# Attention and two feed-forward layers on one core: sums of pv, weight stores, key/query preparations and weight splits at other places of their slots, and four landing buffers for the second layer's weights

## What is computed

```python
scores = q @ k.T / 8                    # 4 batches, 8 heads, 576 positions, dimension 64
attn = softmax(scores, only the 32 largest of each row kept)
x = (attn @ v), laid out as 2304 tokens x 512
h = x @ w_in;   g = h if h >= 1, 0 if h <= -1, else (h + 1)**2 / 4;   x = g @ w_out   # layer 1
h = x @ w_in2;  out = (relu(h) ** 2) @ w_out2                                        # layer 2
```

## Time and profile before

| what | value |
|---|---|
| median of three runs | 1256.47 us |
| the profiled execution | 1258.67 us |
| its span | 1256.9 us |
| TensorE busy | 1191.6 us (95%) |
| VectorE, ScalarE, GpSimd busy | 850.7, 799.0, 745.1 us |
| mean granted TensorE clock | 0.978 of 2.4 GHz |

### The profile page before, as it was taken

One profiled execution on the slowest core, in us unless ns is written; L12 is line 12 of the kernel. 1 busy time (PEld: TensorE's weight loads), 2 busy tenths in 40 slices (PEclk: granted clock), 3 DMA queues, 4 the chain that ended last, 5 costly groups with the idle time before them and its releaser, 6 DMA issues.

```text
span 1256.9 us, 24445 instructions
## 1 busy us (share of the span) xinstructions
PE 1191.6 (95%) x8760; PEld 1128.9 (90%) x8760; DVE 850.7 (68%) x1884; ACT 799.0 (64%) x1788; POOL 745.1 (59%) x620
## 2 busy tenths in 40 slices
PE   6787899999989999999999999999999999999998
PEld 3676889998889999999999999999999999999997
DVE  7999899999888799999999987868730111110000
ACT  7887666776656676776767665666554665554443
POOL 6767787768877767767766766656652222222222
PEclk9958999999999999999999999999999999999999
DMA  6765978567879943244358831456349300870000
GB/s 246 281 246 209 350 274 300 195 249 261 289 267 364 390 153 106 100 136 142 127 168 306 291 126 41 146 178 207 104 147 368 147 35 4 310 290 18 18 17 17
DMA packets 94920, 239.53 MB, mean 191 GB/s; under 512 B 7760, under 2 KB 46672, under 8 KB 82512
## 3 DMA queue, kind: packets, MB, share of 16 engines
q1 hardware_dynamic: 94800, 237.98, 53.2%
HBM read 166.12 MB, written 71.83 MB: 189 GB/s over the span
## 4 chain that ended last, share of the span: by engine, by line
PE 72%; POOL 10%; DVE 6%; ACT 5%; issue 4%; DMA 1%; SPq 1%; ACTq 0%; POOLq 0%
PE h_ps L613 21%; PE y_ps L634 14%; PE y_ps L628 13%; PE score_ps L613 6%; PE pv_ps L572 6%; PE tr_ps L545 4%; POOL s_sb L1087 3%; PE score_ps L510 3%; POOL prob L1092 3%; DVE top L920 2%; DVE rest L922 2%; POOL kq_lo L1070 2%; POOL w_out L1078 1%; PE pv_ps L584 1%; POOL g_lo L1105 1%
## 5 line engine op out<-in xcount | busy, mean ns | idle before, releaser
L1105 POOL TENSOR_TENSOR g_lo<-rg,g_hi 128x256 fp32r<-128x256 f32 x288 | 213.5, 741 | 438.3 <-ACT g_hi L823 231.8
L613 PE MATMUL h_ps<-xt_hi,w_in 128*128 128x256 f32 x1880 | 392.9, 292 | 1.5 <-ACT rg L810 0.9
L613 PEld LDWEIGHTS h_ps<-xt_hi,w_in 128*128 128x128 f32 x1880 | 311.3, 192 | 3.6 <-ACT rg L810 1.1
L920 DVE MAX8 top<-rest 128x8 f32<-128x576 f32 x432 | 304.4, 745 | 0.4
L613 PE MATMUL h_ps<-xt_lo,w_in 128*128 128x256 f32 x940 | 267.1, 284 | 0.0
L1087 POOL TENSOR_SCALAR s_sb<-s_sb,top 128x576 f32<-128x576 f32 x126 | 224.9, 1785 | 16.6 <-DVE top L920 16.6
L628 PE MATMUL y_ps<-g_hi,w_out 128*128 128x256 f32 x1152 | 231.7, 284 | 1.0 <-ACT ys L789 0.7
L922 DVE MATCH_REPLACE8 rest<-top,rest 128x576 f32<-128x576 f32 x288 | 211.5, 741 | 0.0
L634 PE MATMUL y_ps<-w_out,g_hi 128*128 128x512 f32 x576 | 203.6, 395 | 3.8 <-DVE w_out L1004 3.1
L1092 POOL TENSOR_TENSOR prob<-s_sb,prob 128x576 f32<-128x576 f32 x128 | 183.4, 1435 | 14.7 <-ACT s_sb L749 3.9
L628 PEld LDWEIGHTS y_ps<-g_hi,w_out 128*128 128x128 f32 x1152 | 189.6, 192 | 2.2 <-issue 1.0
(11 more groups left out here) (90 smaller groups left out, 2077.0 us busy)
## 6 DMA issues: line engine op xcount, KB each, us to landing
w_in<-w_scratch SPq DMA_DIRECT2D x32, 1024.0 KB, 6.8
w_out<-w_scratch SPq DMA_DIRECT2D x32, 1024.0 KB, 8.1
ks<-kq_scratch SPq DMA_DIRECT2D x46, 576.0 KB, 6.1
qs<-kq_scratch SPq DMA_DIRECT2D x152, 128.0 KB, 4.2
w_scratch<-w_in SPq DMA_DIRECT2D x16, 1024.0 KB, 8.4
w_scratch<-w_out SPq DMA_DIRECT2D x16, 1024.0 KB, 8.3
v_sb<-in_vv_dram SPq DMA_DIRECT2D x48, 325.0 KB, 6.0
stage<-in_w_dram SPq DMA_DIRECT2D x24, 512.0 KB, 4.7
```

What stands on the lines that cost most here:

```text
L613: last = pe.matmul(h_bank(k), wi[:, f // 2, w, m, cols], x[:, m, :], start=(m == 0 and n == 0), stop=(m == KT - 1 and n == 2))
L920: dve.max(best, src[:, :]).then_inc(rank_step, 1)
L1105: pool.tensor_tensor(g_lo[k % 2][:, :], g_sb[k % 2][:, :], g_hi[k % 2][:, :].bitcast(F32), ALU.subtract).then_inc(g_lo_done, 1)
```

## The change

It edits where things stand in their slots, and the landing buffers:

- The sums of pv stand two operations late in slots 4 to 8 too (`n < SIGNED`, which is 9).
- Preparations: slot 10 becomes 9, 17 becomes 18, and 28, 30, 32 become 29, 31, 33. For slots 10 to 17 (`SINGLE`; these are 12 and 15) ScalarE's kq_hi stands at the head of its slot.
- Layer 1's blocks are stored in slots 10 to 20 instead of 10 to 17.
- Layer 2's blocks: slots 19 to 28 take 1, 1, 1, 2, 2, 2, 2, 2, 2, 1 of them (before: 1, 2, 2, 1, 2, 2, 1, 2, 2, 1). ScalarE's high part stands at the head of the slot (`split_second`), VectorE's low part behind op 2 and activate(3n). Block 17 goes from VectorE to GpSimd, where the low part stands at the slot's end as before.
- Landing: four buffers, `stage[0]`, `stage[1]`, and the idle kq_lo and kq_hi. Block i is loaded when block i - 4 is split. The kq buffers are taken after the restack of the ninth preparation (slot 18), and the tenth (slot 29) waits until all 32 blocks are split.
- In slots 18 to 22 (`DEFERRED`) activate(3n + 2) goes behind both(0) of the next slot. From slot 18 on activate(3n + 1) stands in front of op 4 instead of behind it.
- ScalarE's `hi_at(q)` stands behind the exponential of t = 1 in every slot.

```diff
--- before.py
+++ after.py
@@ -32,17 +32,20 @@
 SIGNED = 9
 PREPS = BATCH * PAIRS
 PREP_ORDER = (2, 3, 0, 1, 4, 5, 6, 7, 8, 9, 10, 11, 12, 13, 14, 15)
-PREP_SLOT = (-1, 1, 3, 5, 7, 10, 12, 15, 17, 28, 30, 32, 38, 41, 44, 47)
+PREP_SLOT = (-1, 1, 3, 5, 7, 9, 12, 15, 18, 29, 31, 33, 38, 41, 44, 47)
+IDLE_KQ = sum(s < 19 for s in PREP_SLOT)
+SINGLE = range(10, 18)
+DEFERRED = range(18, 23)
 WBLOCKS = 16
 W_ORDER = [("in", 0)] + [x for j in range(7) for x in (("in", j + 1), ("out", j))] + [("out", 7)]
 W1_SLOT = [-1, 0, 0, 1, 2, 2, 3, 4, 4, 5, 6, 6, 7, 8, 8, 9]
-W2_PER_SLOT = (1, 2, 2, 1, 2, 2, 1, 2, 2, 1)
+W2_PER_SLOT = (1, 1, 1, 2, 2, 2, 2, 2, 2, 1)
 W_SLOT = W1_SLOT + \
          [19 + s for s, c in enumerate(W2_PER_SLOT) for _ in range(c)]
 
 
 STAGE_SLOT = [-1, -1, -1, -1] + [max(s, 0) for s in W_SLOT[0:12]] + [s - 1 for s in W_SLOT[16:]]
-STORE_SLOT = [10 + i // 2 if i < WBLOCKS else W_SLOT[i] + 1
+STORE_SLOT = [10 + 2 * i // 3 if i < WBLOCKS else W_SLOT[i] + 1
               for i in range(2 * WBLOCKS)]
 JOBS = [(1, 0), (1, 1), (2, 0), (2, 1), (1, 2), (1, 3), (1, 4), (1, 5), (2, 2), (2, 3), (2, 4), (2, 5),
         (1, 6), (1, 7), (1, 8), (2, 6), (2, 7), (2, 8)]
@@ -126,17 +129,12 @@
 
 def by_vector(i):
 
-    return i >= WBLOCKS and i % 2 == 1
+    return i >= WBLOCKS + 3 and i % 2 == 1
 
 
 def stage_at(i):
 
-    return i % 4 if i < WBLOCKS else i % 2
-
-
-def staged_count(i):
-
-    return i // 4 + 1 if i < WBLOCKS else WBLOCKS // 4 + (i - WBLOCKS) // 2 + 1
+    return i % 4
 
 
 def own_bank(k):
@@ -294,7 +292,9 @@
 
         def stage_of(i):
 
-            return (stage[0], stage[1], xr, ys)[stage_at(i)]
+            if i < WBLOCKS or stage_at(i) < 2:
+                return (stage[0], stage[1], xr, ys)[stage_at(i)][:, :]
+            return (kq_lo, kq_hi)[stage_at(i) - 2][:, 0:2 * MODEL].bitcast(F32)
 
         def h_bank(k):
 
@@ -321,6 +321,9 @@
                 g = PREP_ORDER[at]
                 if at:
                     sp.wait_ge(restacked, 16 * 3 * at)
+                if at == IDLE_KQ:
+                    for i in range(2):
+                        sp.wait_ge(w_lo_done[i], WBLOCKS)
                 sp.dma_start(kq_lo[:, :].bitcast(F32), kq[g // PAIRS, g % PAIRS]).then_inc(kq_loaded, 16)
 
             def restack(at):
@@ -378,11 +381,11 @@
                     load_v(e // PAIRS, e % PAIRS, e % 2)
 
             def stage_block(i):
-                if i >= WBLOCKS:
-                    sp.wait_ge(w_lo_done[i % 2], i // 2)
-                elif i >= 4:
+                if i >= 4:
                     sp.wait_ge(w_lo_done[i % 2], i // 2 - 1)
-                sp.dma_start(stage_of(i)[:, :], w_raw[i]).then_inc(w_staged[stage_at(i)], 16)
+                if i >= WBLOCKS and stage_at(i) >= 2:
+                    sp.wait_ge(restacked, 16 * 3 * IDLE_KQ)
+                sp.dma_start(stage_of(i), w_raw[i]).then_inc(w_staged[stage_at(i)], 16)
 
             def store_block(i):
                 sp.wait_ge(w_lo_done[i % 2], i // 2 + 1)
@@ -687,11 +690,11 @@
 
             def split_w(i):
                 s, b = i // WBLOCKS, i % WBLOCKS
-                act.wait_ge(w_staged[stage_at(i)], 16 * staged_count(i))
+                act.wait_ge(w_staged[stage_at(i)], 16 * (i // 4 + 1))
                 if s:
                     wait_block_free(act, s, b)
                     act.wait_ge(w_moved[b], 16)
-                act.activation(w_block(b)[:, 0, :], stage_of(i)[:, :], ACT.Copy).then_inc(w_hi_done, 1)
+                act.activation(w_block(b)[:, 0, :], stage_of(i), ACT.Copy).then_inc(w_hi_done, 1)
 
             def copy_scores(n, t):
                 u = 2 * n + t
@@ -845,7 +848,12 @@
                         copy_x(c)
 
             def split_new(n):
-                if n in PREP_SLOT:
+                if n in PREP_SLOT and n not in SINGLE:
+                    split_kq(PREP_SLOT.index(n))
+
+            def split_second(n):
+
+                if n in PREP_SLOT and n in SINGLE:
                     split_kq(PREP_SLOT.index(n))
                 for i in range(WBLOCKS, 2 * WBLOCKS):
                     if W_SLOT[i] == n:
@@ -864,7 +872,12 @@
                     for t in range(2):
                         keep_by_sign(n - 1, t)
                 x_at(n)
-                hi_at(q - 1)
+                if n - 1 in DEFERRED:
+                    split_second(n)
+                    hi_at(q - 1)
+                else:
+                    hi_at(q - 1)
+                    split_second(n)
                 curve_at(q)
                 if here:
                     negate(n)
@@ -874,11 +887,11 @@
                 if before:
                     copy_main(n - 1, 0)
                 copy_at(q)
-                hi_at(q)
                 if q < UP_POS[0]:
                     split_new(n)
                 if here:
                     exponentiate(n, 1)
+                hi_at(q)
                 curve_at(q + 1)
                 if nxt:
                     copy_scores(n + 1, 1)
@@ -1001,7 +1014,7 @@
                 dve.wait_ge(w_hi_done, i + 1)
                 dve.wait_ge(w_lo_done[i % 2], i // 2)
                 b = w_block(i % WBLOCKS)
-                dve.tensor_tensor(b[:, 1, :], stage_of(i)[:, :], b[:, 0, :].bitcast(F32),
+                dve.tensor_tensor(b[:, 1, :], stage_of(i), b[:, 0, :].bitcast(F32),
                                   ALU.subtract).then_inc(w_lo_done[i % 2], 1)
 
             def split_handed(c):
@@ -1024,6 +1037,8 @@
                         rank(n, 1, op)
 
                 both(0)
+                if n - 1 in DEFERRED:
+                    activate_at(3 * n - 1)
                 if n in (NORMAL, NORMAL + 1):
                     clear_corners(n)
                 both(1)
@@ -1031,7 +1046,7 @@
                     if n == x_slot(c) + 1:
                         split_handed(c)
                 read_at(3 * n)
-                behind = 2 if n < RAW_SLOTS else 1 if n < UP_POS[0] // 3 else 0
+                behind = 2 if n < SIGNED else 1 if n < UP_POS[0] // 3 else 0
                 for op in (2, 3, 4, 5, 6):
                     if past and op == 2 + behind:
                         add_to_total(n - 2)
@@ -1041,16 +1056,19 @@
                         scale_pv(n - 2)
                     if op == 4:
                         read_at(3 * n + 1)
+                        if n >= DEFERRED[0]:
+                            activate_at(3 * n + 1)
                     both(op)
                     if op == 2:
                         activate_at(3 * n)
-                    if op == 4:
+                        for i in range(2 * WBLOCKS):
+                            if W_SLOT[i] == n:
+                                split_w(i)
+                    if op == 4 and n < DEFERRED[0]:
                         activate_at(3 * n + 1)
                 read_at(3 * n + 2)
-                activate_at(3 * n + 2)
-                for i in range(2 * WBLOCKS):
-                    if W_SLOT[i] == n:
-                        split_w(i)
+                if n not in DEFERRED:
+                    activate_at(3 * n + 2)
                 if n - 1 in SOON:
                     add_to_total(n - 1)
                     invert_total(n - 1)
@@ -1075,7 +1093,7 @@
                 if i >= 2:
                     pool.wait_ge(w_lo_done[i % 2], i // 2)
                 b = w_block(i % WBLOCKS)
-                pool.tensor_tensor(b[:, 1, :], stage_of(i)[:, :], b[:, 0, :].bitcast(F32),
+                pool.tensor_tensor(b[:, 1, :], stage_of(i), b[:, 0, :].bitcast(F32),
                                    ALU.subtract).then_inc(w_lo_done[i % 2], 1)
 
             def mask(n, t):
```

## The result

Five runs of the kernel after took 1246.47 to 1249.99 us, median 1248.31; the kernel before 1255.52 beside them. The two medians are 7.2 us apart. The ratio measured for the two kernels is 0.9936 (95% interval 0.9926 to 0.9947), which is 8.0 us (6.7 to 9.3), and I go by it; 13.0 were forecast. The profiled execution is the one of 1248.31 us.

A forecast was written before the change was run, and what follows sets the result against it. TensorE, busy 95% of the 1256.9 us span, was the bound, leaving its idle and half-clock time. -1.2 - 0.7 - 0.3 + 0.65 - 11.4 gave -13.0: 1258.67 to 1245.7, less 2.2 for the median, 1243.5; range 1237 to 1251.5.

The forecast's parts named there:

- rival 1: Slots 22 to 27: VectorE and GpSimd exclude each other (the lock), 4.5 us less gain, -8.5, 1248; chance 0.2.
- (f): Slots 19 to 29, layer 2's splits: earlier high and low parts remove waits, -11.4 us; ends -6.5 and -15.
- SyncE's, "nothing": SyncE's queue: four-buffer waits and spread stores cost nothing; the wait before preparation 29 at worst 2 us once.
- Rival 4: SyncE's queue holds loads, blocks land late, slots 22 to 28 keep their length: about -2 left, 1254.5; chance 0.07.
- (g): hi_at(q) behind the exponential and activate(3n + 1) ahead of op 4: 0 us; ends -1 and +2 for the activation.
- Rival 3: Slots 35 to 56: early activation closes the ranking loop, TensorE waits 1 us each, +9, 1265.5; chance 0.08.
- (c): Slots 12 and 15: early kq_hi removes GpSimd's 0.37 us wait each time, -0.7 us; ends 0 and -2.
- (d): Preparation 17 moved to slot 18, its 2.8 us before another mask: -0.3 us; ends -1 and +0.6.
- (e): Preparations moved to slots 29, 31, 33: one leaves slot 28, so +0.65 us here.
- (a): Slots 4 to 8: later pv sums remove VectorE's waits, -2.7 us at the place; -1.2 together with (b).
- (b): Preparation 10 moved to slot 9: slot 10's mask up to 2.2 us earlier; -1.2 together with (a).
- Rival 2: All at the floor: splits fit without trace, slow clock goes too, about -18, 1238.5; chance 0.15.

The follow-up runs named there:

- experiment 1: Kernel after, with block 16 loaded at the end of SyncE's slot 17 instead of 18: 1244.12 us, ratio 0.9897 to the kernel before.
- Experiment 6: Experiment 2's kernel with ScalarE's high parts and VectorE's low parts of layer 2's blocks back at the slot's end: 1249.90 us.
- experiment 5: Experiment 1's kernel with two landing buffers for layer 2's blocks instead of four, kq buffers unused: 1257.38 us, ratio 1.0007 to the kernel before.
- experiment 2: Kernel after, with SyncE issuing layer 2's block loads ahead of the same slot's stores and loads of x and y: 1242.48 us, ratio 0.988 to before.
- experiment 12: The kernel before, unchanged, run for a second profile: 1256.78 us, span 1255.0.
- experiment 4: Experiment 2's kernel with the ninth preparation back in slot 17 and its high part at the end of ScalarE's slot: 1247.24 us.

## Why the prediction was right, and where it was not

The measured 1248.3 lies in the range, the sign and the main mechanism hold, and the size is 5 us off. It is also rival 1's number, 1248, but not by rival 1's sum: the 5.5 us missing in slots 19 to 29 came back when one load was moved (experiment 1), 2.3 of them by way of the lock. By its own steps:

- **(f), the splits: the mechanism is right, and the sum once block 16 lands in time** (144.2 us forecast for slots 19 to 29, 144.0 in experiment 1, 149.5 in the kernel after). Experiment 6 shows the place in the slot to be worth 7 us, experiment 5 that it needs the buffers. That the sum fits so well is luck: slot 19 keeps 1.6 us where 0.6 was taken, slots 22 to 27 keep 3.0 where 3.9 was, slot 28 keeps 0.7 where nothing was, and of the 0.7 for each of the two jobs that begin, slot 29 shows 0.4 and slot 23 nothing.
- **The step that failed is SyncE's, "nothing"**, with its sentence on the blocks that wait for "a split that is a slot old". I looked at the buffers, and for block 16 the buffer was never the question: what was asked of SyncE earlier was a landing, and its load stood behind y's store. Costing a moved instruction means to look at what it waits for as well; here the 9.2 us between the issue and the high part were gone. It cost 5.5 us in the profile, 4.8 by the differences to before: 2.5 in slot 19, 0.5 in slot 20 and 2.3 in slots 22 and 23, where the low parts then met the masks. Rival 4 had the mechanism, landings that come late, but with other causes and a price of 11 us.
- **(g): right about slots 35 to 56** (281.4 us from slot 34's end to slot 56's before, 280.7 after) **and wrong about slots 22 and 23**: with experiment 2's order of loads the early activation is worth 4.5 us there. The -11.4 of (f) contained this by luck. VectorE's wait before this activation in slots 36 to 38 is 1.4 us, not about 2. Rival 3 fell.
- **(c)** -0.7 became -1.7 to -1.9 (slot 13 from 13.85 and 14.02 to 12.53, slot 16 from 12.96 to 12.53), the far end that took in the slow clock: before had a granted clock of 0.60 from 150 to 154 us behind the wait of the earlier trace rows, the kernel after 1.00. No experiment took this part back by itself, nor the later stores of layer 1's blocks or the place of `hi_at(q)`. **(d)** -0.3 for slot 18 is -1.1; what the preparation does to slot 19, the 1.6 just named, is counted in (f). **(e)** +0.65 is +1.3 (slots 30 to 34).
- **(a) and (b)**: -1.2, not settled (the end of slot 12 lies at 142.9 us on the mean of eleven profiles, 144.1 on that of the two of before, with 3.7 us between the eleven). Slot 11 is 2.1 us shorter in every profile, as (b) says, and slots 3 to 10 vary too much to tell the rest.
- **Rival 1, the lock**, is there: six slots with both halves (22 to 27) are 5.6 us above the floor in the kernel after, 2.3 of them in slots 22 and 23, where the masks are slowed; that lies between my 3.9 and the rival's 8.4. In experiment 2 they are 0.0 to 0.9 above it, 2.9 in all. How much of the 2.9 is the lock was not tried. Rival 2's floor was not reached.
- **A reading of the rows.** The second of the two waits of 1.15 us (340.16 us) is in slot 27 by the pv rows, not in 26; slot 26 has one of 1.14, so nothing hangs on it.
- **The base.** I subtracted 2.2 us for a long execution; experiment 12 puts such a difference into slots 0 to 13, whose stalls differ from execution to execution, so it hardly touched (c) to (g).

## What to carry over

When an instruction is moved to an earlier place, trace what it waits for back to the queue that issues it: a load is as early as the last thing in front of it in its queue, not as its buffer is free, and its landing is no constant (4.6 to 10.5 us for the load of block 16; the longest had the most traffic ahead of it, which is read from the profiles and was not tried by itself). At the head of an engine that works in order one late landing can cost more than itself (5.04 us of wait on ScalarE, 5.5 us in eleven slots) or less (5.85 us of wait in experiment 4, where slot 19 is 4.6 above the floor and the slots behind it are not touched): it depends on where the operations of the next slots then fall. And before a place in a slot is called free, look at which operation of the other engine it will fall on.

## What was not expected of the hardware

How much VectorE and GpSimd slow each other depends on the operation and on the start. VectorE's 1.21 us low part of a block has two inputs in SBUF, GpSimd's mask is one tensor and a number for each row. If the low part starts 0.2 us into the 1.73 us mask, the mask takes 2.94 (269.79 against 269.57); if it starts 0.95 us in (267.42 against 266.47), the mask takes 1.73, VectorE still 1.21, and the next operation 1.65 for its usual 1.43. The fourteen profiles of this case together show this: with a start 0.61 to 0.95 us into a mask (20 times) neither operation is slowed, though GpSimd's next one can be, as above. With 0.22 to 0.41 us the mask takes 2.94 to 3.14 in ten of the cases; in four others, 0.13 to 0.41 us in, it takes 1.73 to 2.00 and VectorE 1.55 to 1.70. Of four starts 1.1 us in, all in the two profiles of before, two slow the mask to 2.7. GpSimd's multiplication (1.43 us, two inputs in SBUF) is different: when VectorE starts 0.04 to 0.29 us into it, GpSimd is not slowed, and VectorE takes 2.23 to 2.48, nearly its own time and the rest of the multiplication; in the two cases that start within 0.03 us of each other it is GpSimd that takes 2.5.

The rule of the Trainium skill's page "SBUF — State Buffer", section "SBUF: two separate sides", which the prediction cites, also says that the operation that starts first has the shared ports for its whole duration and the second waits. The multiplication agrees with it. The mask does not: by the recorded starts it is the first that pays (2.94 is 1.73 and 1.21), and from 0.61 to 0.95 us in the two overlap, 0.8 us in the case shown, and neither pays for it. What in the mask decides this was not tried.
